# Pooling the values on VectorE instead of GpSimd, with the second raw half in another tile

## The reference

```python
q_d = q.reshape(B, H, Sd, 4, D).mean(axis=3)      # k_d, v_d alike
out = np.repeat(sm_attn(q_d, k_d, v_d), 4, axis=2) + local_attention(q, k, v, reach=3)
x = out.transpose(0, 2, 1, 3).reshape(B, S, 512)
u = x + real(fft(fft(x, axis=1), axis=2))
u2 = u + relu(norm(u) @ w_ch1) @ w_ch2
y = (sigmoid(causal_conv5(u2)) * (u2 @ w_val)) @ w_out
```

## Time and profile before

| what | us |
|---|---|
| median of three runs | 796.44 |
| the profiled execution's own time | 796.44 |
| its span, first to last instruction | 794.7 |
| TensorE busy | 736.6 (93%) |
| VectorE busy | 386.1 (49%) |
| ScalarE busy | 192.9 (24%) |
| GpSimd busy | 152.6 (19%) |

### The profile page before, as it was taken

The page is one execution under the profiler, slowest core; times in us unless marked ns, Lnnn a source line. Parts: engine busy times, 40 slices in busy tenths (PEclk is TensorE's granted clock), DMA queues, the critical chain, the costliest instruction groups (busy, mean ns, idle before and its releaser), DMA issues.

```text
span 794.7 us, 15623 instructions
## 1 busy us (share of the span) xinstructions
PE 736.6 (93%) x5960; PEld 547.2 (69%) x5960; DVE 386.1 (49%) x925; ACT 192.9 (24%) x417; POOL 152.6 (19%) x130
## 2 busy tenths in 40 slices
PE   2758958999999998999999998999999999999998
PEld 2634546777767776777767676777776677777776
DVE  4446684543643862543653871543553771113552
ACT  1634531222212121222212122222212121111101
POOL 8001677981101311000101221000200300000000
PEclk9999957999999999999999999999999999999999
DMA  9993228022000136022000127022000000000001
GB/s 261 294 256 81 67 100 192 17 64 63 10 1 32 38 84 177 2 57 65 14 1 31 31 65 198 6 54 64 18 1 1 1 30 31 1 1 1 2 15 45
DMA packets 42096, 49.07 MB, mean 62 GB/s; under 512 B 4784, under 2 KB 35568, under 8 KB 40944
## 3 DMA queue, kind: packets, MB, share of 16 engines
q1 hardware_dynamic: 32608, 31.06, 15.7%
q10 hardware_dynamic: 9424, 17.06, 6.9%
HBM read 43.38 MB, written 4.72 MB: 61 GB/s over the span
## 4 chain that ended last, share of the span: by engine, by line
PE 79%; DVE 7%; SPq 5%; issue 3%; POOL 3%; DMA 3%; ACT 0%; DVEq 0%; POOLq 0%
PE P L546 24%; PE Y L563 22%; PE P L676 4%; PE Y L676 4%; PE Y L665 4%; PE A L572 4%; SPq L421 3%; DVE prob_or_un L1065 2%; SPq L425 2%; PE A L533 2%; PE A L455 2%; PE A L526 2%; DMA kl<-qk_win 2%; PE A L516 2%; PE A L626 1%
## 5 line engine op out<-in xcount | busy, mean ns | idle before, releaser
L546 PE MATMUL P<-unT,w_wv 128*128 128x288 f16 x1536 | 215.6, 293 | 5.4 <-issue 4.7
L563 PE MATMUL Y<-hT,w 128*128 128x288 f16 x1536 | 215.2, 287 | 1.5 <-DVE xT L1121 1.5
L1100 DVE SCALAR_TENSOR_TENSOR hT<-P,hT 128x288 f16<-128x288 f32 x128 | 58.6, 458 | 290.4 <-ACT hT L786 290.4
L546 PEld LDWEIGHTS P<-unT,w_wv 128*128 128x128 f16 x1536 | 150.6, 100 | 52.2 <-issue 12.3
L563 PEld LDWEIGHTS Y<-hT,w 128*128 128x128 f16 x1536 | 144.7, 98 | 45.9 <-issue 7.0
L786 ACT ACTIVATE hT<-P 128x288 f16<-128x288 f32 x128 | 52.4, 410 | 202.5 <-PE P L546 202.4
L1136 DVE SCALAR_TENSOR_TENSOR gate<-xT,cw,gate 128x288 f32<-128x288 f32 x128 | 66.4, 519 | 4.5
L757 ACT ACTIVATE prob_or_un<-prob_or_un 73x288 f32<-73x288 f32 (+1 forms) x52 | 23.3, 448 | 121.6 <-DVE prob_or_un L973 121.6
L1255 POOL MEMSET x<- 1x512 f32 x4 | 2.1, 516 | 219.9 <-ACT x L775 219.9
L311 POOL TENSOR_TENSOR x<-x,fb 128x256 f32<-128x256 f32 (+1 forms) x12 | 12.1, 1006 | 116.8 <-DVE fb L1041 116.8
L676 PE MATMUL P<-shared,wo 128*128 128x288 f32 x128 | 32.1, 410 | 0.7 <-DVE shared L1146 0.5
(11 more groups left out here) (162 smaller groups left out, 868.0 us busy)
## 6 DMA issues: line engine op xcount, KB each, us to landing
kl<-qk_win SPq DMA_DIRECT2D x38, 140.0 KB, 6.7
ql<-qk_win SPq DMA_DIRECT2D x19, 256.0 KB, 6.8
vl<-v_win SPq DMA_DIRECT2D x72, 65.0 KB
pair_or_folded<-qk_pool SPq DMA_DIRECT2D x8, 580.0 KB, 6.1
pair_or_spectrum<-qk_pool SPq DMA_DIRECT2D x8, 580.0 KB, 6.7
out<-ot ACTq DMA_DIRECT2D x32, 144.0 KB, 1.8
w_wv<-w_ch ACTq DMA_DIRECT2D x4, 1024.0 KB, 11.6
w<-w_ch ACTq DMA_DIRECT2D x4, 1024.0 KB, 12.5
```

Of the source, the lines that this page charges most:

```text
L546: last = mm(P[s % 2][:, 0:HN], w1s(k, f, wt), unT[:, ut, k, ha * HN:(ha + 1) * HN], start=k == 0 and wt + ut == 0, stop=k == KD - 1 and wt ...
L563: last = mm(Y[d][:, 0:HN], w2s(f, d, wt), hT[s % 3][:, ht, :], start=f == 0 and wt + ht == 0, stop=f == KF - 1 and wt == 1)
L1100: nc.vector.scalar_tensor_tensor(out=hT[s % 3][:, 1, :], in0=P[s % 2][:, 0:HN], scalar=0.0, in1=hT[s % 3][:, 0, :], op0=ALU.max, op1=ALU.s ...
```

## The change

`vraw` names the two places of the raw halves: half 0 stays in `x`, half 1 is now always in `shared`. The probabilities after the transpose get tiles of their own (`probT0`, `probT1`), and `prob_or_un` is half as large. The load of half 0 waits as before. The load of half 1 waits for `step_over` and is issued after qk pair 3, ahead of the windows. From batch 1 on VectorE does the pooling, one `tensor_reduce` over four rows per half: half 0 behind the two `pool_qk` at the start of the loop step, half 1 in slot 2, behind `unit_shift`. GpSimd's pooling stays for batch 0 alone. The subtraction of unit 0 waits for `unT_ps` instead of `v_pooled`. GpSimd's `second_weights` 1 to 7 all stand at the end of its opening step. `gated(m, 0, 0)` waits for the pooling of both halves, which is done earlier on the same engine.

```diff
-        prob_or_un = sb("prob_or_un", [128, 4 * DM])
+        prob_or_un = sb("prob_or_un", [128, 2 * DM])
-        probT = [prob_or_un[:, DM * i:DM * (i + 1)] for i in range(2, 4)]
+        probT = [sb(f"probT{i}", [128, 512]) for i in range(2)]
+        vraw = [x[0:GP, 0:4, :], shared[0:GP, :].rearrange("p (r c) -> p r c", r=4)]
...
-        POOLING = {3: 2, 5: 3}
+        POOLING = {2: [("v", 1)], 3: [("qk", 2)], 5: [("qk", 3)]}
...
             def load_v(b, k):
                 if later(b):
-                    sp.wait_ge(uT_ps if k == 0 else unT_ps, 6 * b)
+                    if k == 0:
+                        sp.wait_ge(uT_ps, 6 * b)
+                    else:
+                        sp.wait_ge(step_over, b)
...
                 load_pair(b, 1)
-                if later(b):
-                    load_v(b, 1)
                 load_v(b, 0)
...
                 load_pair(b, 3)
+                if later(b):
+                    load_v(b, 1)
...
+            def pool_v(b, k):
+                dve.wait_ge(ld_vraw[k], 16 * (b + 1))
+                nc.vector.tensor_reduce(vd[:, k, :, 0:D], vraw[k].rearrange("p r (h c) -> p h c r", h=H), axis=AX.X,
+                                        op=ALU.add).then_inc(v_pooled, 1)
...
                 if u == 0 and later(b):
-                    dve.wait_ge(v_pooled, 2 * b + 1)
+                    dve.wait_ge(unT_ps, 6 * b)
...
                     if m is not None:
                         pool_qk(b, 1)
+                        pool_v(b, 0)
...
-            def step(b):
-                if later(b):
-                    pool_v(b, 1)
-                    pool_v(b, 0)
-                if isinstance(b, int) and b == 1:
-                    for c in range(2, WCH):
-                        second_weights(c)
-                    pool.wait_ge(w2_split, WCH)
+            def step(b, first=False):
                 zero_rows(b)
...
-                if opening(b):
-                    second_weights(1)
+                if first:
+                    for c in range(1, WCH):
+                        second_weights(c)
+                    pool.wait_ge(w2_split, WCH)
```

More of the change, by code:

```diff
@@ L128, in fused_kernel @@
         rstd = sb("rstd", [128, 3, 2])
-        un = [prob_or_un[:, DM * i:DM * (i + 1)] for i in range(4)]
+        un = [prob_or_un[:, DM * i:DM * (i + 1)] for i in range(2)] + [p[:] for p in probT]
         xT = sb("xT", [128, KD, TAPS - 1 + N])
@@ L240, in fused_kernel @@
         CONV_AT = [22, 24, 26, 28]
-        POOLING = {3: 2, 5: 3}
-        POOLING_FIRST = {1: 1, 3: 2, 5: 3}
+        POOLING = {2: [("v", 1)], 3: [("qk", 2)], 5: [("qk", 3)]}
+        POOLING_FIRST = {1: [("qk", 1)], 3: [("qk", 2)], 5: [("qk", 3)]}
         WEIGHT_LOADS = {2: [0], 3: [1], 4: [2], 5: [3], 7: [4], 8: [5], 11: [8, 6], 12: [7]}
@@ L262, in banks @@
             return A[0], A[1], A[1]
[L264 to L268, removed]
         def values(b, t):
@@ L362, in load_v @@
                 if later(b):
-                    sp.wait_ge(uT_ps if k == 0 else unT_ps, 6 * b)
+                    if k == 0:
+                        sp.wait_ge(uT_ps, 6 * b)
+                    else:
+                        sp.wait_ge(step_over, b)
                     sp.sem_inc(passed, 1)
-                sp.dma_start(raw_values(b, k), v_pool[b, k]).then_inc(ld_vraw[k], 16)
+                sp.dma_start(vraw[k], v_pool[b, k]).then_inc(ld_vraw[k], 16)
             def attend_loads(b):
@@ L1137, in conv, with gated @@
                                                        op0=ALU.mult, op1=ALU.add).then_inc(tap_done, 1)
-            def gated(b, ha, d):
+            def gated(b, ha, d, attending):
                 n = 8 * b + 4 * ha + d
+                if attending and ha == 0 and d == 0:
+                    dve.wait_ge(v_pooled, 2 * (b + 2))
                 dve.wait_ge(val_ps, n + 1)
@@ L1167, in step @@
                                 unit_scale(b, u)
-                        if s in (POOLING if m is not None else POOLING_FIRST):
-                            pool_qk(b, (POOLING if m is not None else POOLING_FIRST)[s])
+                        for what, k in (POOLING if m is not None else POOLING_FIRST).get(s, []):
+                            if what == "qk":
+                                pool_qk(b, k)
+                            else:
+                                pool_v(b, k)
                         for u in unit_at(b, m, s, LAG_AV + 1):
@@ L1203, in step @@
                     for d in range(KD):
-                        gated(m, 0, d)
+                        gated(m, 0, d, False)
                     for d in range(KD):
@@ L1207, in step @@
                     for d in range(KD):
-                        gated(m, 1, d)
+                        gated(m, 1, d, False)
                 else:
@@ L1212, in step @@
                     combine(b, 2)
-                    gated(m, 0, 0)
+                    gated(m, 0, 0, True)
                     statistics(b, 1)
-                    gated(m, 0, 1)
+                    gated(m, 0, 1, True)
                     normalise(b, 1)
@@ L1218, in step @@
                     columns(b, 1)
-                    gated(m, 0, 2)
-                    gated(m, 0, 3)
+                    gated(m, 0, 2, True)
+                    gated(m, 0, 3, True)
                     statistics(b, 2)
@@ L1231, in step @@
                     for d in range(KD):
-                        gated(m, 1, d)
+                        gated(m, 1, d, True)
             for k in kl:
@@ L1297, in step, with first_values @@
                     inv_std(b, j)
-                if opening(b):
-                    second_weights(1)
-            def pool_v(b, k):
-                half = raw_values(b, k).rearrange("p (h r) c -> p h r c", h=2)
-                pool.wait_ge(ld_vraw[k], 16 * (b + 1))
+                if first:
+                    for c in range(1, WCH):
+                        second_weights(c)
+                    pool.wait_ge(w2_split, WCH)
+            def first_values(k):
+                half = vraw[k].rearrange("p (h r) c -> p h r c", h=2)
+                pool.wait_ge(ld_vraw[k], 16)
                 pt(half[:, 0], half[:, 0], half[:, 1], ALU.add).then_inc(v_half, 1)
-                pool.wait_ge(v_half, 2 * b + (k if opening(b) else 1 - k) + 1)
+                pool.wait_ge(v_half, k + 1)
                 pt(vd[:, k, :, 0:D], half[:, 0, 0].rearrange("p (h c) -> p h c", h=H), half[:, 0, 1].rearrange("p (h c) -> p h c", h=H),
@@ L1327, in _ @@
             nc.gpsimd.memset(spread[:], 0.0).then_inc(spread_made, 1)
-            pool_v(0, 0)
-            pool_v(0, 1)
+            first_values(0)
+            first_values(1)
             pool.wait_ge(v_pooled, 2)
@@ L1337, in _ @@
             pool.wait_ge(quartered, 2)
[L1338 to L1341, removed]
+            step(0, first=True)
+            with pool.Fori(0, B - 1) as it:
+                step(it + 1)
 def kernel(**inputs):
```

## The result

The changed kernel takes 802.29 us (median of 7 runs, 799.42 to 803.4) against 796.44 (median of 7 runs beside them, 795.72 to 799.62). Eleven more executions, the profiled one among them, lie between 797.5 and 803.74, and the median of all 18 is 800.8. The ratio over all runs is 1.0054, interval 1.0034 to 1.0076: it is slower by 0.54%, some 4.3 us, and lies outside the forecast range. The two medians of 7 are further apart, 5.85 us. The profiled execution took 802.28 us with a span of 800.5 (before: 796.44 and 794.7).

A forecast was written before the change was run, and what follows sets the result against it. TensorE, busy 93% of the span, was taken as the bound, so other engines' work costs only where TensorE waits. Sum: 796.44 + 0.3 (first loop step) - 0.45 (jump back) = 796.3 us, break-even at 0.53; range 792.2 to 798.8.

The forecast's parts named there:

- the price of the reduction: VectorE's pooling of one half, 2048 elements a partition: 2.27 us, bounds 2.1 and 4.54, scaled from two shorter reductions.
- The first pause: First loop step, before `mlp_up(2)`: TensorE idle 2.1 us for half 0's load and pooling, replacing a 1.77 us wait.
- The wait at the scores of unit 1: First loop step: TensorE's 1.77 us idle before these scores goes, replaced by the 2.1 us pause; net +0.3 us.
- Cost: nothing: Half 1 pooled in slot 2: later steps' `hidden_low(3)` 0.55 us later, pooled product and next scores still in time.
- in slot 2 it hurts only from about 5 us: Strided-sum rival: a reduction in slot 2 delays TensorE only once it takes about 5 us.
- One fall before and one after: 0: First loop step: TensorE's clock falls once behind the new pause as behind the old, so no net cost.
- The jump back: TensorE's pauses of 2.59 and 2.14 us at the loop's jump: emptier queues save 0.45 us, once.
- the rival with the emptier queues: Rival B, chance 0.24: both jump-back pauses fall to about 1.29 us; time given as 792.5 us.
- Half 1: Load for slot 2: landing 130.8 in the first step; later issued at 307.1, landing 312.4 to 313.1, before VectorE comes.
- that rival: Rival D, chance 0.06: half 1 lands past 316.8, too late for slot 2; 798.3 us with 1 us beyond.
- the strided sum: Rival C, chance 0.13: each reduction takes 4.54 us, its surplus on the path in the first loop step; 798.6 us.
- the signs of being wrong: Reductions above 3 us, VectorE idle before vd<-shared, jumps under 1.5 us with clock 1.00, or TensorE waits in slots 3 to 5.

The follow-up runs named there:

- contig: Changed kernel with raw values of batches 1 to 3 laid out so the reduction reads neighbouring floats, local attention built from rearranged rows; 797.06 us, ratio 1.0007.
- contig2: Changed kernel with the same contiguous layout for the reduction, but the windows of the local attention left as they were; 796.59 us, ratio 0.9997.
- probe: Kernel before the change, with ten extra VectorE instructions in the last step: seven reductions at distances 1 to 512 floats, three additions; one execution, 797.69 us.
- act_order: Changed kernel with ScalarE copying the transposed probabilities of unit u - 2 ahead of the exponential of unit u; 799.08 us, ratio 1.0033.
- late_v0: Changed kernel with VectorE's pooling of half 0 moved to slot 1, behind the shift of unit 0; 810.66 us, ratio 1.0184.
- tt_adds: Changed kernel with VectorE summing each raw half in two additions of contiguous rows instead of one strided reduction; 799.01 us, ratio 1.0018.

## Why the prediction was wrong, point by point

Two steps failed. **The first failed step is the price of the reduction**, "So 2.27 is my value", taken from two contiguous reductions and an addition that jumps. It measures 3.66 and 3.75 us. The bounds (2.1 and 4.54) held it, the choice inside them did not. The 2.27 itself was exact for contiguous data (2.27 to 2.28 in contig, contig2 and probe); the fault was to read L311 as "strided" when it goes between two places and the reduction goes round four. contig2 shows that the loss hangs on this price: with reductions of 2.27 us the ratio is 0.9997, as forecast. But the true price put into the forecast's own sum gives 796.3 + 1.4 = 797.7, still inside the range. It takes the second failed step, below, to explain where the time went: the path on which the price reaches TensorE from slot 2.

**The first pause.** Forecast: 2.1 us, of which the landing 5.71 after issue (measured 5.71) and the reduction 2.27. Measured 3.75, longer by 1.65, of which 1.4 is the reduction. The rest is that TensorE reached the place 0.3 us sooner (5.6 us into the step instead of 5.9), since the first low stretch of its clock ended sooner. Same mechanism, a term mis-sized. The wait at the scores of unit 1 went, as forecast.

**The second failed step is "Cost: nothing" for half 1 in slot 2**, and with it "in slot 2 it hurts only from about 5 us". It is a path left out, not a size. I followed the delayed shift to its first user on TensorE and found it in time, which it was. I did not follow it through ScalarE, whose exponential of unit 2 stands ahead of the copy of unit 0. With 3.7 us it cost 0.62, 0.58 and 0.58 us; with 2.27 (contig, contig2) nothing. act_order shows the cause: with the copy ahead of the exponential the three waits are gone at the same price. The border thus lies between 2.27 and 3.73 us.

**The clock.** "One fall before and one after: 0" was right in number. The low stretch at the longer pause lasted twice as long, 6.8 instead of 3.4 us, but 2.1 us of it fell into the pause, and the first stretch of the step happened to end 0.8 us sooner; the net is some +0.25 us. That the net is small is partly luck.

**The jump back.** -0.45 was taken for emptier queues. The pauses are 2.31 and 2.22 us (before 2.59 and 2.14), 0.2 less together. The stretch of the first pause was indeed emptier (DMA share 0.67 at 306 to 308 after, 1.09 at 302 to 304 before), and over the seven kernels made from the changed one, all of which hold the windows back in the same way, the pauses ran from 2.34 to 3.06 at the first jump and from 1.96 to 2.18 at the second. In probe, whose loads go out as in the kernel before, they are 2.35 and 2.06. The difference between the changed kernel and the one before (0.28 and 0.08) is thus no larger than that between two executions of the same steps (0.24 and 0.08) by more than a few hundredths. Nothing here shows that emptier queues shorten the pauses, so the rival with the emptier queues falls, and my term has nothing under it.

**Half 1.** It was issued at 311.05, 2.21 us into its step (forecast 307.1, 2.53 into it), and had landed when VectorE came for it: that rival falls as well. In the first loop step the landing forecast at 130.8 was early: the sum divides by 196 GB/s, where the earlier trace rows also have 170. In late_v0, where VectorE waited for it, half 1 landed 13.2 us into the step (forecast 11.3). VectorE came later too, 15.6 us into it in the changed kernel and 13.6 in contig2, so nothing was lost. Half 0 of the later steps, the weight pieces and the later windows cost nothing, as forecast; contig2's second and third steps bear this out.

**The rival that was right** is the strided sum. Its time, 798.6 for 4.54 us a piece, counted the first loop step alone, so even at a price above the true one it stays under the measured time. At the measured price its own arithmetic gives 797.7. The timed runs want 796.44 x 1.0054 = 800.7. The missing 3 us are ScalarE's order (1.8), the jump term that did not come (0.25), the clock (0.25), the rest of the first pause (0.25), and some 0.45 that I can't assign. The profiled execution lies another 1.5 us higher through its opening. Whether that also lifts the median of the seven runs, 802.29, no trace shows.

**The spread.** The range took the runs of a kernel to lie within 1.0 us of each other, after three runs. The 29 runs of the kernel before lie between 792.77 and 801.02. Of the signs of being wrong that the prediction names, two came: reductions above 3 us, and a wait of TensorE in slots 3 to 5.

## What to carry to other kernels

Price a reduction by the pattern of its reads: when its groups are spread over four places at least 16 bytes apart, lay out the data so that they lie together, or take two contiguous additions where GpSimd is not at work at the same time. When a delayed instruction is found to be in time for its user, look also at what stands behind its consumer on every in-order engine between them; here the late unit 2 cost unit 0. And before work is moved to another engine, try an earlier load: it removed the wait (0.9947) that the move only exchanged for others (1.0054).

## What the runs showed of the hardware that I had not expected

- A fp32 reduction of 72 x 2048 in groups of four takes 2.27 us with members 1 or 2 floats apart and 3.65 to 3.77 us with 4 to 512 floats; no distance tried gave a value between (3 was not tried).
- An addition whose second input alternates between two distant places costs no more than a contiguous one (1.23 against 1.21 us); with four places it takes 1.95.
- TensorE's pause at the loop's jump back is 1.96 to 3.06 us over the ten profiled kernels, no shorter where the queues are emptier. At or behind it the granted clock falls to 0.50 for some 3.4 us in 17 of the 20 cases. The other three had no such fall: the third step of act_order took 176.55 us against 178.2 in most others, the second of tt_adds 178.89 against 180.3 to 180.5, and the third of late_v0 is the last.
- In the first slots of a loop step the low clock lasted 3.4 us with waits of 1.77, 2.19 and 2.46 us (before, probe, contig2) and 6.8 us with waits of 3.23 to 3.75 us. It is no matter of the wait's length alone: with a wait of 2.36 us it lasted 6.8 us in the second step of late_v0, and with the same wait in the third it did not fall.
